# Unread TensorE products of an attention stage: 512 bf16 columns each, further ones ahead of the turns of x and the first scores, masks' products on 128 rows

## The reference

```python
q_d, k_d, v_d = mean over groups of 4 positions            # "pooled": 144 positions
out_up   = repeat(softmax(scale * q_d @ k_d.T) @ v_d, 4)
mask     = abs(pos[:, None] - pos[None, :]) < 4            # "local": a band of 7
out_local = softmax(where(mask, scale * q @ k.T, -1e9)) @ v
x = (out_up + out_local) as 2304 rows of 512
```

## Time and profile before

| | |
|---|---|
| median of 3 runs | 1020.61 us (1017.17 to 1022.37) |
| the profiled execution, its own time | 998.79 us |
| its span in the trace | 997.0 us |
| mean granted TensorE clock of the profiled execution | 0.952 |
| TensorE busy (matmuls) | 901.7 us, 90% |
| VectorE, ScalarE, GpSimd busy | 641.3, 341.5, 319.0 us |

### The profile page before, as it was taken

The page is one execution under the profiler, slowest core; times in us unless marked ns, Lnnn a source line. Parts: engine busy times, 40 slices in busy tenths (PEclk is TensorE's granted clock), DMA queues, the critical chain, the costliest instruction groups (busy, mean ns, idle before and its releaser), DMA issues.

```text
span 997.0 us, 22961 instructions
## 1 busy us (share of the span) xinstructions
PE 901.7 (90%) x8236; PEld 846.3 (85%) x8236; DVE 641.3 (64%) x1674; ACT 341.5 (34%) x1065; POOL 319.0 (32%) x306
## 2 busy tenths in 40 slices
PE   7999999822799999999999999999999999999995
PEld 6777878721689988998898899889988998999995
DVE  4395766577689857765776577567657765772342
ACT  2667687630343142133114311421241133115211
POOL 4464554300440253036014502530261045015201
PEclk9599999955799999999999999999999999999998
DMA  7766541153352320212212021202121121212000
GB/s 162 166 143 166 129 115 42 34 143 101 103 159 75 97 67 25 86 46 79 78 38 81 27 84 34 74 24 84 45 79 52 49 77 46 84 29 80 25 1 24
DMA packets 122497, 76.02 MB, mean 76 GB/s; under 512 B 64328, under 2 KB 105288, under 8 KB 122440
## 3 DMA queue, kind: packets, MB, share of 16 engines
q1 hardware_dynamic: 119368, 65.83, 24.1%
q0 software_dynamic: 3072, 9.44, 3.3%
HBM read 65.81 MB, written 9.44 MB: 75 GB/s over the span
## 4 chain that ended last, share of the span: by engine, by line
PE 55%; issue 16%; DVE 15%; POOL 7%; ACT 3%; DMA 2%; SPq 2%; DVEq 0%; POOLq 0%; ACTq 0%
PE banks L872 14%; PE banks L874 12%; PE banks L873 12%; DVE onehot L1098 5%; POOL w1s L1395 4%; PE banks L883 3%; ACT prob L513 2%; DVE place L1095 2%; POOL turning L1403 2%; PE banks L304 2%; SPq L198 2%; PE banks L255 2%; PE banks L267 1%; DVE place L1096 1%; PE banks L356 1%
## 5 line engine op out<-in xcount | busy, mean ns | idle before, releaser
L1362 ACT CAST hid<-act 128x288 fp32r<-128x288 f32 x128 | 55.4, 433 | 341.9 <-DVE act L1195 338.0
L872 PE MATMUL banks<-xy,win 128*128 128x288 f32 x512 | 153.8, 300 | 8.3 <-DVE xy L1186 8.3
L872 PE MATMUL banks<-hid,wout 128*128 128x288 f32 x512 | 155.1, 303 | 0.0
L874 PE MATMUL banks<-hid,wout 128*128 128x288 f32 x512 | 152.7, 298 | 0.0
L873 PE MATMUL banks<-xy,win 128*128 128x288 f32 x512 | 151.4, 296 | 0.0
L873 PE MATMUL banks<-hid,wout 128*128 128x288 f32 x512 | 151.2, 295 | 0.0
L874 PE MATMUL banks<-xy,win 128*128 128x288 f32 x512 | 150.7, 294 | 0.0
L1403 POOL DMA_INDIRECT turning<-x_rows,id_new x24 | 22.6, 942 | 353.8 <-DVE id_new L1169 349.0
L1193 DVE TENSOR_SCALAR neg<-banks,alph 128x288 f32<-128x288 f32 x128 | 66.2, 517 | 97.6 <-PE banks L874 93.7
L1395 POOL TENSOR_TENSOR w1s<-raw,w1s 128x512 fp32r<-128x512 f32 x62 | 85.9, 1386 | 133.2 <-ACT w1s L1330 133.2
L872 PEld LDWEIGHTS banks<-xy,win 128*128 128x128 f32 x512 | 96.3, 188 | 10.8 <-DVE xy L1186 8.5
(11 more groups left out here) (184 smaller groups left out, 2021.2 us busy)
## 6 DMA issues: line engine op xcount, KB each, us to landing
raw<-in_moe_w SPq DMA_DIRECT2D x128, 256.0 KB, 3.1
qn<-in_q SPq DMA_DIRECT2D x48, 96.0 KB, 2.4
kn<-in_k SPq DMA_DIRECT2D x48, 96.0 KB, 2.4
vn<-in_v SPq DMA_DIRECT2D x4, 1152.0 KB
x_rows<-xs SPq DMA_DIRECT2D x24, 192.0 KB, 2.1
raw<-in_moe_w_in SPq DMA_DIRECT2D x16, 256.0 KB, 3.6
raw<-in_moe_w_out SPq DMA_DIRECT2D x16, 256.0 KB, 3.6
vw<-in_v SPq DMA_DIRECT2D x16, 204.0 KB
```

The source lines that it names most:

```text
L872: nc.tensor.matmul(out_ap, a_hi, b_hi, start=start, stop=False)
L874: return nc.tensor.matmul(out_ap, a_hi, b_lo, start=False, stop=stop)
L1362: nc.scalar.copy(hid[:, (FC + j) % 3, 0, :], act[:, j % 2, :]).then_inc(h_hi, 1)
```

## The change

A tile `dense`, 128 by 512 in bf16 and all ones, is set by VectorE's first instruction. `pe_fill` now multiplies 128 of its columns by all 512, so each unread product has 512 bf16 columns. The start has 24 of them and waits for `dense` instead of the identities. The unread product in a unit of batch 0 goes to bank 7 and stands ahead of the bank's wait. Three new ones stand ahead of each of the scores 0 to 3 (`LAG` is 3), and one ahead of each turn of x, behind the bank's wait and ahead of the wait for the sum. The masks' tile and `ident16` get 128 rows, so that the masks' products have 128 rows and 128 output rows instead of 96. In the diff, lines of the kernel that stay are shown for place.

```diff
-    mask = sb("mask", [T, 3, 4, W], BF16)
+    mask = sb("mask", [128, 3, 4, W], BF16)
+    dense = sb("dense", [128, 512], BF16)
...
+    pIdle = psum[:, 512 * 7:512 * 8]
...
-        e.wait_ge(pads_made, 4)
+        e.wait_ge(pads_made, 5)
         load_windows(e, 0)
...
         for _ in range(n):
-            nc.tensor.matmul(bank[:, 0:128], ident[:], ident[:], start=True, stop=True)
+            nc.tensor.matmul(bank, dense[:, 0:128], dense[:], start=True, stop=True)
...
             e.wait_ge(qk_in[hp // (HP // 2)], 16 * 2 * R * (b + 1))
+        if b == 0:
+            pe_fill(pIdle, 1)
         pe_bank_free(e, "qk", b, unit)
         bank = pF[PLAN.place["qk", b, unit] % RING]
-        if b == 0:
-            pe_fill(bank, 1)
...
         bank = pS[u % 2]
+        if u <= LAG:
+            pe_fill(pIdle, 3)
         if u >= 2:
             e.wait_ge(exped, u - 1)
...
-                nc.tensor.matmul(bank[0:T, g, 0:4 * W], ident16[0:T, 0:T],
+                nc.tensor.matmul(bank[:, g, 0:4 * W], ident16[:],
...
         pe_bank_free(e, "flip_x", u, 0)
+        bank = pF[PLAN.place["flip_x", u, 0] % RING]
+        pe_fill(bank, 1)
         e.wait_ge(summed, b * NT + x + 1)
-        bank = pF[PLAN.place["flip_x", u, 0] % RING]
...
     def tensor(e):
+        e.wait_ge(pads_made, 1)
+        pe_fill(pIdle, 24)
         e.wait_ge(consts["made"], consts["n_made"])
-        pe_fill(pF[0], 18)
...
     def vector(e):
+        nc.vector.memset(dense[:], 1.0).then_inc(pads_made, 1)
...
     def scalar(e):
-        e.wait_ge(pads_made, 2)
+        e.wait_ge(pads_made, 3)
...
-        ident16 = lasting("ident16", [T, T], BF16)
+        ident16 = lasting("ident16", [128, 128], BF16)
```

## The result

The changed kernel takes 1032.45 us (median of 4 runs, 1031.1 to 1038.38) against 1018.89 for the kernel before in the same set of runs (1016.34 to 1022.37). The ratio is 1.0276, with a 95% interval from 1.0216 to 1.0336. The kernel before scatters by up to 3.6% within one set of runs (998.4 to 1034.74 us in the widest), and the four runs of the changed one by 0.7%, so the two figures can differ.

A forecast was written before the change was run, and what follows sets the result against it. Bound by TensorE's granted clock, falling to half twice in attention, and by busy TensorE mid-batch. Terms -2.3 - 1.0 + 4.3 - 1.4 = -0.4 gave 998.4 us for the profiled execution; likeliest median 1001 us, range 992 to 1024.

The forecast's parts named there:

- The 21.8 us: Timed median over profiled execution (998.79 us): held likelier than not to be longer half-clock stretches in attention, some 47 us more.
- case 3: Rival, chance 0.20: the timed runs' extra 21.8 us are not the clock, so only the summed terms count; 1020 us.
- case 1: Rival, chance 0.42: timed runs have more half-clock stretches, and the change keeps the clock through nearly all attention; 1001 us.
- case 2: Rival, chance 0.13: clock kept in part; at turns of x the product stands behind the bank's wait; 1008 to 1015 us.
- The first fall avoided, -2.3 us: Attention, 25 to 49 us: filled idle stretches keep the clock full; a late load lets at most 2.35 us through.
- The gate of 54.55 us: Attention: GpSimd's wait for batch 1's `vn` load keeps item 6's first half from being ready before 54.55 us.
- The second fall avoided, -1.0 us: Attention, 127 to 130 us: three microseconds at half clock go, saving 1.0 us, bounds 0 and 1.4.
- The price of an unread product, 0.27 us: TensorE at full clock: masks' products of 408 columns, scaled to 512, give 0.27 us per new product where nothing covers it.
- The 24 at the turns of x, +4.3 us: Attention: one new product at each turn, 16 of 24 counted as uncovered, 0.27 us each; bounds 0 and 6.5.
- The start: Kernel's beginning: 24 unread products start about a microsecond earlier, take 7 to 9 us, up to 1 us late; no own term.
- Case 4: Rival, chance 0.13: the new kind moves the throttle no more than the old, falls stay, costs are added; 1023 us.
- Case 5: Rival, chance 0.12: slower; all 24 products at turns of x lie on the path, the clock gains nothing; 1027 us.

The follow-up runs named there:

- after_pad: The changed kernel plus 88 TensorE instructions that only raise an unused semaphore, ahead of the expert loop; 1013.29 us against 1015.12 for the kernel before.
- before_pad: The kernel before plus 168 TensorE instructions that only raise an unused semaphore, ahead of the expert loop; 1059.36 us against 1015.12 for the kernel before.
- before_again: The kernel before with no edit, run again for a second profile; that profile took 1019.39 us.
- after_fit: The changed kernel plus 44 tiny unread products at the end of TensorE's part of attention; 1005.85 us, ratio 0.9983 to the kernel before.
- fit_noturn: after_fit without the 24 unread products at the turns of x and with 68 tiny products; 1005.31 us, ratio 1.0029 to the kernel before.
- kind_alone: The kernel before with only the kind of its 74 unread products changed, plus 74 tiny products at attention's end; 1006.65 us, ratio 1.0007.
- before_104: The kernel before plus 52 tiny unread products (104 instructions) ahead of the expert loop; 1032.96 us, one execution.
- before_120: The kernel before plus 60 tiny unread products (120 instructions) ahead of the expert loop; 1017.90 us, one execution.

## Why the prediction was wrong

**The step that failed** is the sum's silent assumption that behind attention nothing changes. The prediction says that "the sum alone counts" where the clock isn't the cause, and gives the expert passes no term. They took 27.8 us more in the profile and some 22 to 26 us in the medians (after_pad and before_pad), which is more than the whole result. It came from the instruction stream: 88 instructions fewer ahead of the loop moved it from seven 16 KB steps to eight.

**The 21.8 us** were read rightly. I had them as some 47 us more at half clock; before_again shows 48 us more, 22 us longer, with the same passes behind. So the condition of case 3 doesn't hold. What I drew from it, case 1 with 1001 us and a range of 992 to 1008, came true in number only, and only with the loop in its place (1005.85 in after_fit). Its condition, the clock kept through nearly all of attention, did not: after_fit's profile has three stretches at half, 37.5 us together, more than the 27 of before's first profile. That is case 2's mechanism, at a lower time than I gave it.

**The first fall avoided, -2.3 us,** was right about the fall and wrong about what follows. The clock held at 24 us as foreseen, but fell after the next idle stretch, at 29 us. The gate of 54.55 us was the right place, though the load came later: the wait for it grew to 13.10 us, as foreseen (over 10), but the flip stood at 57.59 us, not near 54.6. I priced the gate as a ceiling of the gain only. I didn't ask what TensorE does while it waits there: it stood for 6.57 us, the clock fell, and 19 us of work ran at half. With a longer third stretch that made attention 11.95 us longer in the profiles, against a first profile that was one of before's best executions.

**The second fall avoided, -1.0 us:** not seen. In the changed profile it is longer, from 134.8 to 145.1 us (3.4 us before), behind waits of 0.61 us for a ring bank and 0.51 us for `pdT`. At the first of them the new product stands behind the wait, as case 2 had it.

**The price of an unread product, 0.27 us,** measured 0.22; the estimate of 0.216 that I took from the Trainium skill ("TensorE: Matmul & The Clock Gate", section "Wait — 56ns, not 53.3ns?") and set aside was right. So the old ones became 0.10 us cheaper, not 0.05, and an item of batch 1 is 0.1 us longer where I had 0.2. The 24 at the turns of x, +4.3 us, showed 0.5 us in the medians (after_fit less fit_noturn), cost and clock together.

**The start** went as worked out: the 24 took 7.10 us from 1.56 us on, and the first product behind the first data began at 9.27 us. **Case 4,** that the kind of product moves nothing, is not refuted: kind_alone's first fall stays, and its ratio of 1.0007 (0.9964 to 1.0051) shows no difference. The falls as a whole did not stay, since with the new number and places the first one moved. **Case 5** had the right sign by the wrong way.

Open: why executions of one kernel differ so much in when the clock falls, what exactly sets the instruction that begins a step, and why the price of an eighth step ranges from 15 to 28 us.

## What to carry to other kernels

Count the instructions ahead of a loop and in it whenever an edit adds or removes some on the same engine, even in another stage; a row of the instruction queue whose packets grow is the sign. A transfer that holds back a faster engine can cost more than the gain it swallows: here the clock fell in the wait (6.57 us), and 19 us of work behind it ran at half. Take a profile of one execution for what it is: here the one at hand was 13 to 20 us better than the kernel's medians in the four sets of runs.

## What the runs showed of the hardware

- A loop of 1632 TensorE instructions ran without an instruction packet if it lay in seven steps of 256 instructions (passes of 92.1 us), and fetched nine packets of 16 KB a pass if it lay in eight, at 2 to 6 us a pass (after, before_pad, before_104, before_120).
- An instruction on TensorE that only raises a semaphore took about 0.15 us (12.96 us of wait behind 88, 25.48 behind 168). A tiny product with its weight load took about 0.03 us: 44 of them shortened the wait of 6.21 us to 5.01, and 74 to 4.13.
- TensorE busy for 33.4 of 34 us with small float32 products stayed at 1.2 GHz throughout.
